# Attention, mixture of experts and feed-forward in one kernel: the gate's logits move out of attention

## The chip, the cores and the metric

The kernel runs on one core of a Trainium2 chip. The metric is the device time of one execution in microseconds (us). TensorE is called PE, its weight loads PEld, VectorE DVE, ScalarE ACT, GpSimd POOL and SyncE SP, as in the profile.

## What is computed

Attention over 4 batches of 8 heads, 576 tokens, head size 64, in a window of 128 tokens with a bias by distance; its output, 2304 tokens of 512, goes through a mixture of 8 experts whose shares come from a gate, and then through a leaky feed-forward layer. The part that matters here:

```python
scores = np.where(mask, scale * (q @ k.T) + bias, -1e9)
attn = exp(scores - max); attn = attn / (sum(attn) + 1e-9); x = attn @ v
logits = x @ w_gate                        # [2304, 512] @ [512, 8]
P = exp(logits - logits.max())             # then 8 rounds of row and column scaling
out += P[:, e:e + 1] * (relu(x @ w1[e]) @ w2[e])
```

## The kernel before

**Attention** works on one pair of heads at a time, 16 pairs (`ITERS`), numbered i; two pairs' buffers alternate (`s`). The 576 query tokens of a pair are 4 tiles of 128 and one of 64, worked on in three groups (`GROUPS`): group 0 is tiles 0 and 1, group 1 tiles 2 and 3, group 2 the tile of 64. Each query tile sees at most two key tiles. For each group:

- PE makes the scores (`scores`, L1116), in fp32: each matmul is two PE instructions.
- DVE adds the bias and takes the row maxima (`bias_scores`, L776).
- ACT takes the exponentials and their row sums (`exponentials`, L541).
- DVE adds a small constant to the sums (L786), takes reciprocals (L788) and scales the rows (L792): `normalise`.
- PE transposes the result (`transpose_p`, L1124), ACT copies it from PSUM (`copy_pt`, L550, L551, L556), PE multiplies with the values (`values`, L1146), and ACT copies the pair's output into `x_raw` (`copy_out`, L562, L563).

The order on each engine is written out by hand in `step`, and the groups of neighbouring pairs are interleaved. For step i:

| Engine | Order in step i |
|---|---|
| PE | scores (i, 2); values (i-1, 1); transposes (i, 0); scores (i+1, 0); values (i-1, 2); transposes (i, 1); scores (i+1, 1); values (i, 0); logits; transposes (i, 2) |
| ACT | copy (i-1, 1); exponentials (i, 1); copy (i-1, 2); copy (i, 0); exponentials (i, 2); output copy (i-1); exponentials (i+1, 0) |
| DVE | bias (i, 2); normalise (i, 1); bias (i+1, 0); normalise (i, 2); bias (i+1, 1); normalise (i+1, 0) |
| POOL | splits of weights and of the first operands, in pieces that wait for given scores (`at`, L382 to L480) |

**Logits** (`logits`, L1152 to L1161): tokens are stationary and the gate's weights, 8 columns, are streamed. The 2304 tokens are 20 parts of 128 or 64 tokens; each takes 4 matmuls (8 instructions), one for each 128 of the 512 input dimensions, accumulated in PSUM. 15 parts are made in steps 4 to 15 of attention (one a step, two in steps 7, 11 and 15), 5 in unit 0.

**Units.** The experts and the feed-forward layer are worked through in granules; each granule is two units (k), of 2 x 256 and 2 x 320 tokens. A unit makes seven products of 6 matmuls each (`product`, L1205 to L1208) into three PSUM banks, which ACT copies and DVE combines, and the down products of tiles of the granule before (`down`). In units 0 and 1 the second unit's first operands are still being cast by ACT (`casts`) and split by DVE (`first_lows`). The logits reach `gate` in unit 1 (`gating`), and the shares are made from them in the units that follow.

Of the kernel before, what the change touches and what calls it, by code (L numbers as in the profile page):

```python
# [5 lines left out]
def attention_moe_ffn(nc, qk_t, v_t, w_gate, w_up, w_down, out, shape):  # L6
# [5 lines left out]
    fp32, f32r = mybir.dt.float32, mybir.dt.float32r  # L12
# [22 lines left out]
    STATS = 2 * SLOTS  # L35
    QT = S // P
# [14 lines left out]
    with ctx:  # L51
# [37 lines left out]
        wg = place("wg", KD * E)  # L89
# [21 lines left out]
        assert at[0] <= acc1_end  # L111
        xs = []
# [11 lines left out]
        bank = [ctx.enter_context(nc.psum_tensor(f"bank{i}", [P, 512], fp32)) for i in range(8)]  # L124
        b_s, b_tail, b_p, b_o = (bank[0:2], bank[3:5]), bank[2], bank[5:7], bank[7]
        b_a, b_b, b_c, b_y, b_m = (bank[0], bank[1]), bank[7], (bank[3], bank[4]), (bank[5], bank[6]), bank[2]
        MAXT, NEGM, COLS = 160, 300, 304
# [9 lines left out]
        wg_ready = sem("wg_ready")  # L137
# [26 lines left out]
        def segments(g, s):  # L164


            sc0, st0 = s * SLOTS * 512, s * STATS
            if g == GROUPS - 1:
                nk = P + TAIL
                return [(hd, QT, (QT - 1) * P, nk, 0, sc0 + 2 * g * 512 + hd * nk, st0 + 4 * g + hd) for hd in range(2)]  # L170
            got = []
            for n in range(2):
                t = 2 * g + n
                nk, c = (P, 0) if t == 0 else (2 * P, (2 * P if g else P) * n)
                for hd in range(2):
                    slot = 2 * g + hd
                    got.append((hd, t, max(t - 1, 0) * P, nk, c, sc0 + slot * 512 + c, st0 + 2 * slot + n))
            return got
# [57 lines left out]
        def logits_at(tile):  # L236

            return tile * E if tile < 16 else 7 * TAIL + (tile - 16) * E
# [10 lines left out]
        def _(sp):  # L249
# [37 lines left out]
            sp.dma_start(wg[:, :].rearrange("p (k e) -> p k e", e=E),  # L287
# [244 lines left out]
        def _(act):  # L532
# [12 lines left out]
            def copy_pt(i, g, s):  # L545
# [76 lines left out]

            def early_copies(k, u):
# [3 lines left out]
                a.activation(t1[:, 0:n], b_a[u][:, 0:n], ACT.Copy).then_inc(t1_copied, 1)  # L627
                act.wait_ge(c_done, 2 * k + 1)
# [24 lines left out]
            def unit(k, u, x2=(), phase=None):  # L653

                n = NU[u]
                early_copies(k, u)
                casts(phase, k, 0)
                copy_u2(k, u)
                act.wait_ge(c11_done, k + 1)
                a.activation(hs_hi[u][:, hidden_part(u, 0, 0)], b_b[:, 0:n], ACT.Relu).then_inc(hi_done, 1)  # L660
                casts(phase, k, 1)
                for tile in x2[0:1]:
                    copy_x2(tile)
                act.wait_ge(c22_done, k + 1)
                a.activation(hs_hi[u][:, hidden_part(u, 1, 1)], b_c[1 - u][:, 0:n], ACT.Relu).then_inc(hi_done, 1)  # L665
                act.wait_ge(c12_done, k + 1)
# [3 lines left out]
                a.activation(hs_hi[u][:, hidden_part(u, 0, 1)], b_a[u][:, 0:n], ACT.Relu).then_inc(hi_done, 1)  # L670
                casts(phase, k, 3)
# [87 lines left out]
        def _(dve):  # L759
            d = nc.vector  # L760

            dve.wait_ge(rel_ready, 1)
# [19 lines left out]
            def normalise(i, g, s):  # L782
                rows = rows_of(g)
                st = slice(s * STATS + 4 * g, s * STATS + 4 * g + len(segments(g, s)))
                dve.wait_ge(exp_done, GROUPS * i + g + 1)
                d.tensor_scalar_add(esum_eps[0:rows, st], esum[0:rows, st], EPS).then_inc(eps_added, 1)  # L786
                dve.wait_ge(eps_added, GROUPS * i + g + 1)
                d.reciprocal(einv[0:rows, st], esum_eps[0:rows, st]).then_inc(inv_done, 1)  # L788
                dve.wait_ge(inv_done, GROUPS * i + g + 1)
# [3 lines left out]
                last.then_inc(normed, 1)  # L793

# [13 lines left out]
            def step(i, s, pair, last=False):  # L808
# [15 lines left out]
            bias_scores(0, 1, 0, 0)  # L824
            normalise(0, 0, 0)
# [82 lines left out]
            def gating(k, point):  # L908
# [3 lines left out]
                if k == 1 and point == 0:  # L912
                    dve.wait_ge(lg_done, 1)
                    split = 16 * E
                    d.tensor_copy(gate[:, 0:split], b_m[:, 0:split]).then_inc(gate_in, 1)
                    d.tensor_copy(gate[:, split:], b_m[:, 7 * TAIL:7 * TAIL + 2 * TILES * E - split]).then_inc(gate_in, 1)
                    dve.wait_ge(gate_in, 2)
# [183 lines left out]
        def _(pe):  # L1101
# [25 lines left out]
            def values(i, g, s, first=False):  # L1127
# [12 lines left out]
                for n, (hd, t, kt, nk, _, b, to) in enumerate(todo):  # L1140
                    if n == len(todo) - 1 and g == 0:

                        pe.wait_ge(normed, GROUPS * i + 3)
# [8 lines left out]
            def logits(b, n):  # L1152

                tile, _, t, rows, p0 = [(tile, *part) for tile in range(TILES) for part in token_parts(tile)
                                        if part[0] == b % 2][n]
                c = logits_at(b // 2 * TILES + tile)
                for kd in range(KD):
                    x = b * HALF + kd * S + t
                    last = m.matmul(b_tail[p0:p0 + rows, c:c + E], x_raw[:, x:x + rows],  # L1159
                                    wg[:, kd * E:(kd + 1) * E], start=kd == 0, stop=kd == KD - 1)  # L1160
                return last  # L1161

# [239 lines left out]
```

## Time and profile before

| | us |
|---|---|
| median of 3 runs | 2050.15 (2049.0 to 2050.66) |
| the profiled execution | 2049.61 |
| its span | 2047.8 |
| end of attention on PE | 137.64 |
| PE busy / PEld busy | 2032.2 / 1815.3 |
| DVE / ACT / POOL busy | 1183.9 / 643.1 / 1167.4 |

The mean granted clock of TensorE is 0.999 of full speed. Some 93% of the span is units; attention is the first 7%. Times in the rows are microseconds from the span's start. In a timeline each row is one instruction or several like it in a row (x8): start, time, engine, line, operation, names, shapes, and in brackets the idle time ahead of it and what ended it. A record of PE, DVE or ACT can overlap the start of the next instruction, so the cost of one in a queue is read from start to start.

### The profile page before, as it was taken

What the parts mean: (1) busy time and instruction counts of PE and PEld (TensorE: products, weight loads), DVE (VectorE), ACT (ScalarE), POOL (GpSimd) and SP (SyncE); (2) the same over time, 40 slices, a digit from 0 to 9 for tenths busy, and PEclk for the clock granted to TensorE, in tenths of its full rate; (3) what the DMA queues carried; (4) which work ended last, traced back from release to release, by engine and by line L of the source; (5) the groups of instructions that cost most, each with busy time, mean ns of one, the idle gap of its engine ahead of it and who ended that gap; (6) DMA issues with size and microseconds to landing.
All of it is one profiled execution on the core that took longest, in us unless ns stands there. A gap on an engine that the chain in (4) does not pass through costs nothing.

```text
span 2047.8 us, 36400 instructions
## 1 busy us (share of the span) xinstructions
PE 2032.2 (99%) x12475; PEld 1815.3 (89%) x12475; DVE 1183.9 (58%) x2708; ACT 643.1 (31%) x1776; POOL 1167.4 (57%) x1451
## 2 busy tenths in 40 slices
PE   8999999999999999999999999999999999999999
PEld 6788999899999899999999999999999989998998
DVE  8876766555555555564555554554554565667666
ACT  8972222222222222233222222222222244334332
POOL 3425556555566565576555566655555575667551
PEclk9999999999999999999999999999999999999999
DMA  5311111111111111111111111111111111111211
GB/s 178 119 66 42 42 42 41 51 41 51 41 41 41 51 41 51 41 37 47 42 52 41 51 41 41 41 51 41 51 41 41 41 41 52 42 52 56 73 42 47
DMA packets 31311, 104.86 MB, mean 51 GB/s; under 512 B 3968, under 2 KB 4480, under 8 KB 31232
## 3 DMA queue, kind: packets, MB, share of 16 engines
q1 hardware_dynamic: 31232, 103.84, 15.1%
q8 instruction: 45, 0.74, 0.1%
q14 instruction: 34, 0.28, 0.0%
HBM read 99.11 MB, written 4.72 MB: 51 GB/s over the span
## 4 chain that ended last, share of the span: by engine, by line
PE 95%; DVE 2%; POOL 1%; ACT 1%; issue 1%; DMA 0%; SPq 0%; ACTq 0%; DVEq 0%; POOLq 0%
PE bank L1227 16%; PE bank L1228 16%; PE bank L1229 16%; PE bank L1205 14%; PE bank L1208 14%; PE bank L1207 14%; PE bank L1146 1%; PE bank L1124 1%; PE bank L1116 1%; PE bank L1159 1%; ACT sc L541 1%; DVE sc L792 1%; POOL up_lo L369 0%; DVE sc L776 0%; PE bank L1243 0%
## 5 line engine op out<-in xcount | busy, mean ns | idle before, releaser
L876 DVE SCALAR_TENSOR_TENSOR acc<-bank,gate,acc 128x512 f32<-128x512 f32 x495 | 371.6, 751 | 573.8 <-PE bank L1229 573.8
L1205 PE MATMUL bank<-x_hi,up_hi 128*128 128x256 f32 (+1 forms) x2240 | 663.3, 296 | 2.0 <-POOL up_lo L369 1.9
L1208 PE MATMUL bank<-x_hi,up_lo 128*128 128x256 f32 (+1 forms) x2240 | 662.9, 296 | 0.0
L1207 PE MATMUL bank<-x_lo,up_hi 128*128 128x256 f32 (+1 forms) x2240 | 662.3, 296 | 0.0
L1228 PE MATMUL bank<-down_lo,hs_hi 128*128 128x512 f32 x1440 | 568.0, 394 | 0.0
L1227 PE MATMUL bank<-down_hi,hs_hi 128*128 128x512 f32 x1440 | 567.5, 394 | 0.4 <-DVE hs_lo L990 0.4
L1229 PE MATMUL bank<-down_hi,hs_lo 128*128 128x512 f32 x1440 | 560.3, 389 | 0.0
L1205 PEld LDWEIGHTS bank<-x_hi,up_hi 128*128 128x128 f32 x2240 | 423.9, 189 | 30.0 <-POOL up_lo L369 2.7
L1207 PEld LDWEIGHTS bank<-x_lo,up_hi 128*128 128x128 f32 x2240 | 423.9, 189 | 23.6
L1208 PEld LDWEIGHTS bank<-x_hi,up_lo 128*128 128x128 f32 x2240 | 423.8, 189 | 0.0
L369 POOL TENSOR_TENSOR up_lo<-stage_up,up_hi 128x256 fp32r<-128x256 f32 x546 | 384.7, 742 | 6.3
L1229 PEld LDWEIGHTS bank<-down_hi,hs_lo 128*128 128x128 f32 x1440 | 270.7, 188 | 61.6
L358 POOL TENSOR_TENSOR stage_up<-stage_up 128x256 f32<-128x256 f32 x78 | 58.3, 748 | 450.0 <-PE bank L1208 450.0
L1227 PEld LDWEIGHTS bank<-down_hi,hs_hi 128*128 128x128 f32 x1440 | 271.7, 189 | 38.1 <-issue 0.8
L1228 PEld LDWEIGHTS bank<-down_lo,hs_hi 128*128 128x128 f32 x1440 | 271.6, 189 | 32.4
L375 POOL CAST down_hi<-stage_down 128x1024 fp32r<-128x1024 f32 x78 | 81.1, 1039 | 263.5 <-PE bank L1229 263.5
L379 POOL TENSOR_TENSOR down_lo<-stage_down,down_hi 128x256 fp32r<-128x256 f32 x312 | 221.4, 743 | 6.3
L984 DVE SCALAR_TENSOR_TENSOR hs_lo<-bank,hs_hi 128x256 fp32r<-128x256 f32 (+1 forms) x512 | 208.9, 448 | 1.5 <-ACT hs_hi L660 1.1
L865 DVE TENSOR_TENSOR acc<-bank,acc 128x512 f32<-128x512 f32 x153 | 105.5, 689 | 111.1 <-PE bank L1229 109.7
L634 ACT ACTIVATE u<-bank 128x256 f32<-128x256 f32 (+1 forms) x160 | 65.7, 411 | 324.7 <-PE bank L1208 324.7
L627 ACT ACTIVATE t<-bank 128x256 f32<-128x256 f32 (+1 forms) x160 | 65.6, 410 | 304.0 <-PE bank L1208 303.7
L665 ACT ACTIVATE hs_hi<-bank 128x256 fp32r<-128x256 f32 (+1 forms) x128 | 52.6, 411 | 340.0 <-DVE bank L968 340.0
(118 smaller groups left out, 1823.1 us busy)
## 6 DMA issues: line engine op xcount, KB each, us to landing
stage_up<-w_up SPq DMA_DIRECT2D x80, 512.0 KB, 3.4
stage_down<-w_down SPq DMA_DIRECT2D x80, 512.0 KB, 3.4
qk<-qk SPq DMA_DIRECT2D x15, 608.0 KB, 3.8
v_nat<-v SPq DMA_DIRECT2D x16, 320.0 KB, 2.9
result<-acc SPq DMA_DIRECT2D x16, 256.0 KB, 2.6
result<-acc SPq DMA_DIRECT2D x4, 128.0 KB, 3.0
qk<-qk SPq DMA_DIRECT2D x2, 128.0 KB, 2.1
qk<-qk SPq DMA_DIRECT2D x1, 192.0 KB, 2.5
```

The costliest lines, as they stand in the source:

```text
L369: last = g.tensor_tensor(up_lo[s][:, part], raw(op), up_hi[s][:, part], ALU.subtract)
L375: g.tensor_copy(down_hi[s][:, :], stage_down[:, :]).then_inc(w_step, 1)
L379: last = g.tensor_tensor(down_lo[s][:, part], stage_down[:, part], down_hi[s][:, part], ALU.subtract)
L865: last = d.tensor_tensor(to, y[:, :], to, ALU.add)
L876: last = d.scalar_tensor_tensor(out=to, in0=y[:, :], scalar=share(g, tile, e), in1=to, op0=ALU.mult, op1=ALU.add)
L984: d.scalar_tensor_tensor(out=hs_lo[u][:, part], in0=of[:, 0:NU[u]], scalar=0.0, in1=hs_hi[u][:, part], op0=ALU.max, op1=ALU.subtract).then ...
L1205: m.matmul(to[:, 0:n], up_hi[s][:, w], x_hi[u][:, x], start=first and c == 0, stop=False, skip_group_check=True)
L1207: m.matmul(to[:, 0:n], up_hi[s][:, w], x_lo[u][:, x], start=False, stop=False, skip_group_check=True)
L1208: last = m.matmul(to[:, 0:n], up_lo[s][:, w], x_hi[u][:, x], start=False, stop=c == 1, skip_group_check=True)
L1227: m.matmul(to[:, :], hs_hi[u][:, h], down_hi[s][:, w], start=f == 0, stop=False)
L1228: m.matmul(to[:, :], hs_hi[u][:, h], down_lo[s][:, w], start=False, stop=False)
L1229: last = m.matmul(to[:, :], hs_lo[u][:, h], down_hi[s][:, w], start=False, stop=f == 1)
```

## The change

The logits leave attention. In units 0 and 1 they are made in 8 pieces of 256 or 320 tokens: the gate's weights, padded with zeros to 32 columns for each 128 input dimensions, are stationary, the tokens are streamed, and the four matmuls of a piece write to four groups of 32 PSUM partitions. ACT copies the piece to SBUF (`lt_sb`), and a second matmul for each part of tokens, with the piece stationary and a 0/1 matrix (`sel`) streamed, adds the four groups and turns the result to tokens by experts. The calls of `logit_tiles` for a piece follow one product after the piece.

In attention, PE's transposes of group 2 move behind values (i-1, 1) of the next step, ahead of the transposes of group 0. DVE makes bias (i+1, 1) before it normalises group 2, and takes the addition and the reciprocal for group 2 and the next pair's group 0 together (`normalise_two`); for this the statistics have new places. ACT copies both heads' transposes of a group with one instruction. On SP the gate weights' DMA waits for POOL's clearing of `wg`.

```diff
@@ names and places @@
+    STAT_AT = ((2, 6, 10), (12, 16, 0))
...
-        wg = place("wg", KD * E)
+        wg = place("wg", KD * P // 4)
+        sel = place("sel", E)
...
+        at[0] = acc1_at
+        lt_sb = [place(f"lt_sb{n}", NU[1]) for n in range(2)]
...
+        def piece(n):
+            return n // 2, NU[0] * (n % 2), NU[n % 2]
@@ SP and POOL @@
+            sp.wait_ge(wg_clear, 1)
+            sp.dma_start(wg[:, :].rearrange("p (k e) -> p k e", e=P // 4)[:, :, 0:E],
                          w_gate.rearrange("(k p) e -> p k e", p=P)).then_inc(wg_ready, 16)
...
+            g.memset(wg[:, :], 0.0).then_inc(wg_clear, 1)
@@ ACT @@
-                    for hd in range(2):
-                        last = a.activation(pt_sb[:, to + hd * 512:to + hd * 512 + n], b_p[hd][:, 0:n], ACT.Copy)
+                    both = [of.rearrange("p (h c) -> p h c", h=2)[:, :, 0:n]
+                            for of in (pt_sb[:, to:to + 1024], bank56[:, :])]
+                    last = a.activation(*both, ACT.Copy)
...
+            def copy_lt(k, *pieces):
+                for n in pieces if isinstance(k, int) else ():
+                    if n // 7 == k:
+                        act.wait_ge(lt_done, n + 1)
+                        cols = piece(n)[2]
+                        a.activation(lt_sb[n % 2][:, 0:cols], b_m[:, LT:LT + cols], ACT.Copy).then_inc(lt_copied, 1)
...
                 a.activation(t1[:, 0:n], b_a[u][:, 0:n], ACT.Copy).then_inc(t1_copied, 1)
+                copy_lt(k, 0, 7)
...
                 early_copies(k, u)
+                copy_lt(k, 1)
                 casts(phase, k, 0)
+                copy_lt(k, 2)
                 copy_u2(k, u)
+                copy_lt(k, 3)
@@ DVE @@
+            d.memset(esum[:, :], 1.0)
...
+            def normalise_two(i, s, n):
+                dve.wait_ge(exp_done, GROUPS * (i + 1) + 1)
+                inverses(P, STAT_AT[s][2], STAT_AT[s][2] + 6, n)
+                scale(2, s)
+                scale(0, 1 - s)
...
                 bias_scores(i, 2, s, pair)
-                normalise(i, 1, s)
+                normalise(i, 1, s, 2 * i + 1)
                 if last:
                     sums(0, 2)
-                if not last:
+                    normalise(i, 2, s, 2 * i + 2)
+                else:
                     bias_scores(i + 1, 0, 1 - s, after)
-                normalise(i, 2, s)
-                if not last:
                     bias_scores(i + 1, 1, 1 - s, after)
-                    normalise(i + 1, 0, 1 - s)
+                    normalise_two(i, s, 2 * i + 2)
+            dve.wait_ge(ident_ready, 1)
+            d.reduce_sum(sel[:, :], ident[:, :].rearrange("p (j c) -> p c j", c=P // 4)[:, 0:E, :], AX.X
+                         ).then_inc(sel_ready, 1)
@@ PE @@
+            def logits(n):
+                b, t, cols = piece(n)
+                if n == 0:
+                    pe.wait_ge(wg_ready, 16)
+                    pe.wait_ge(o_done, ITERS)
                 for kd in range(KD):
+                    rows = slice(kd * P // 4, (kd + 1) * P // 4)
                     x = b * HALF + kd * S + t
+                    last = m.matmul(b_m[rows, LT:LT + cols], wg[:, rows], x_raw[:, x:x + cols], start=True, stop=True)
+                last.then_inc(lt_done, 1)
+            def logit_tiles(n):
...
+                pe.wait_ge(lt_copied, n + 1)
+                for tile in range(TILES):
+                    for half, t0, rows, p0 in token_parts(tile):
+                        if half == b % 2 and t <= t0 < t + cols:
+                            c = (b // 2 * TILES + tile) * E
+                            last = m.matmul(b_m[p0:p0 + rows, c:c + E], lt_sb[n % 2][:, t0 - t:t0 - t + rows],
+                                            sel[:, :], start=True, stop=True)
+            def logit_work(k, point):
...
+                n = 7 * k + point
+                if 0 < n <= 2 * B:
+                    last = logit_tiles(n - 1)
...
+                if n < 2 * B:
+                    logits(n)
...
                 scores(i, 2, s)
                 if not first:
                     values(i - 1, 1, 1 - s)
+                    pe.wait_ge(normed, GROUPS * i)
+                    transpose_p(2, 1 - s)
...
                 values(i, 0, s, first)
-                if i >= KD:
-                    logits(i // KD - 1, i % KD)
-                    if i % KD == KD - 1:
-                        logits(i // KD - 1, KD)
-                transpose_p(2, s)
...
                 product(a_bank, u, s, A11, B11, True).then_inc(a_done, 1)
+                logit_work(k, 0)
...
                 product(c_bank, u, s, S1, T1, True).then_inc(c_done, 1)
-                if isinstance(k, int) and k == 0:
-                    pe.wait_ge(o_done, ITERS)
-                    logits(B - 1, 0)
+                logit_work(k, 1)
```

`logit_work(k, point)` stands behind each of the seven products of units 0 and 1 in the same way, and the old calls of `logits` in unit 0 are gone.

## Rows read from the trace of the kernel before

**Rows 1.** The page, part 1: busy time and share of the span of each engine.

```profile
PE 2032.2 (99%) x12475; PEld 1815.3 (89%) x12475; DVE 1183.9 (58%) x2708; ACT 643.1 (31%) x1776; POOL 1167.4 (57%) x1451
```

**Rows 2.** Timeline of PE, early and late attention: start us, us, engine line op.

```profile
9.97 0.88 PE L1124 MATMUL bank<-ident,sc 128*128 128x128 f32 x6 [2.35 <-DVE sc L792]
...
17.60 0.88 PE L1124 MATMUL bank<-ident,sc 128*128 128x128 f32 x6 [0.42 <-DVE sc L792]
...
129.76 0.88 PE L1124 MATMUL bank<-ident,sc 128*128 128x128 f32 x6
...
134.32 1.62 PE L1159 MATMUL bank<-wg,x_raw 128*128 128x8 f32 x16
...
137.64 0.39 PE L1205 MATMUL bank<-x_hi,up_hi 128*128 128x256 f32 x1
```

**Rows 3.** Timeline of PE, one step of attention with logits.

```profile
56.22 0.88 PE L1124 MATMUL bank<-ident,sc 128*128 128x128 f32 x6
...
57.88 0.60 PE L1146 MATMUL bank<-pt_sb,v_nat 128*64 128x64 f32 x8
58.41 1.09 PE L1124 MATMUL bank<-ident,sc 128*128 128x128 f32 x8
59.43 1.13 PE L1116 MATMUL bank<-qk 64*128 64x256 f32 x8
60.50 0.88 PE L1146 MATMUL bank<-pt_sb,v_nat 128*64 128x128 f32 x12
61.30 1.06 PE L1159 MATMUL bank<-wg,x_raw 128*128 128x8 f32 x8
...
64.08 0.88 PE L1124 MATMUL bank<-ident,sc 128*128 128x128 f32 x6
```

**Rows 4.** Timeline of DVE, the same step.

```profile
59.50 0.54 DVE L792 TENSOR_SCALAR sc<-sc,einv 64x192 f32<-64x192 f32 x2
60.62 0.42 DVE L776 CUSTOM_DVE_ANT_0 sc<-bank,nbias 128x256 f32<-128x256 f32 x1 [0.58 <-issue]
...
62.00 0.17 DVE L786 TENSOR_SCALAR esum_eps<-esum 128x4 f32<-128x4 f32 x1
...
62.42 1.01 DVE L792 TENSOR_SCALAR sc<-sc,einv 128x128 f32<-128x128 f32 x4
63.35 0.35 DVE L776 CUSTOM_DVE_ANT_0 sc<-bank,nbias 64x192 f32<-64x192 f32 x1
```

**Rows 5.** Timeline of ACT, the same step.

```profile
57.13 0.87 ACT L556 ACTIVATE pt_sb<-bank 128x384 f32<-128x384 f32 x2 [0.47 <-PE bank L1124]
```

**Rows 6.** Timelines of POOL and of DVE, early attention.

```profile
15.92 0.83 POOL L399 CAST up_hi<-stage_up 128x768 fp32r<-128x768 f32 x1
...
16.19 1.36 DVE L792 TENSOR_SCALAR sc<-sc,einv 128x128 f32<-128x128 f32 x4
...
31.39 1.64 DVE L792 TENSOR_SCALAR sc<-sc,einv 128x128 f32<-128x128 f32 x4
```

**Rows 7.** Stretches: us, busy by engine, granted clock, DMA share, GB/s.

```profile
103.00:104.00 1.00, 1.00 (x14) 0.78 (x15) 0.35 (x3) 1.00 (x6) 0.25 (x1) 0.88 0.00 0
104.00:105.00 1.00, 1.00 (x12) 1.00 (x10) 0.93 (x8) 0.17 (x2) 0.36 (x1) 0.50 0.27 54
...
107.00:108.00 1.00, 1.00 (x12) 0.67 (x12) 0.02 (x1) 1.00 (x3) 0.00 (x0) 0.91 0.00 0
```

**Rows 8.** Timeline of PE, unit 0: one group of logits.

```profile
139.18 0.96 PE L1159 MATMUL bank<-wg,x_raw 128*128 128x8 f32 x8
139.99 0.36 PE L1205 MATMUL bank<-x_hi,up_hi 128*128 128x256 f32 x1
140.19 0.28 PE L1207 MATMUL bank<-x_lo,up_hi 128*128 128x256 f32 x1
140.31 0.28 PE L1208 MATMUL bank<-x_hi,up_lo 128*128 128x256 f32 x1
```

**Rows 9.** Timeline of ACT: the last output copy of attention.

```profile
138.41 0.21 ACT L563 ACTIVATE x_raw<-bank 128x64 f32<-128x64 f32 x1
```

More of the change, by code:

```diff
@@ L780, in bias_scores, with inverses, scale @@
                 last.then_inc(biased, 1)
-            def normalise(i, g, s):
-                rows = rows_of(g)
[L784 to L789, printed above, removed]
+            def inverses(rows, st0, ends, n):
+                st = slice(st0, ends)
+                d.tensor_scalar_add(esum_eps[0:rows, st], esum[0:rows, st], EPS).then_inc(eps_added, 1)
+                dve.wait_ge(eps_added, n + 1)
+                d.reciprocal(einv[0:rows, st], esum_eps[0:rows, st]).then_inc(inv_done, 1)
+                dve.wait_ge(inv_done, n + 1)
+            def scale(g, s):
+                rows = rows_of(g)
                 for _, _, _, nk, _, c, st in segments(g, s):
@@ L1150, in values @@
                     last.then_inc(pv_done, 1)
[L1152 to L1156, printed above, removed]
+            def logits(n):
[3 more added lines that the diff above has]
+                    pe.wait_ge(o_done, ITERS)
                 for kd in range(KD):
+                    rows = slice(kd * P // 4, (kd + 1) * P // 4)
                     x = b * HALF + kd * S + t
-                    last = m.matmul(b_tail[p0:p0 + rows, c:c + E], x_raw[:, x:x + rows],
-                                    wg[:, kd * E:(kd + 1) * E], start=kd == 0, stop=kd == KD - 1)
-                return last
+                    last = m.matmul(b_m[rows, LT:LT + cols], wg[:, rows], x_raw[:, x:x + cols], start=True, stop=True)
+                last.then_inc(lt_done, 1)
+            def logit_tiles(n):
+                b, t, cols = piece(n)
+                if n == 0:
+                    pe.wait_ge(sel_ready, 1)
+                pe.wait_ge(lt_copied, n + 1)
[5 more added lines that the diff above has]
+                                            sel[:, :], start=True, stop=True)
+                return last
+            def logit_work(k, point):
+                if not isinstance(k, int):
+                    return
+                n = 7 * k + point
+                if 0 < n <= 2 * B:
+                    last = logit_tiles(n - 1)
+                    if n == 2 * B:
+                        last.then_inc(lg_done, 1)
+                if n < 2 * B:
+                    logits(n)
             def step(i, s, first=False, last=False):
@@ L1302, in unit @@
                 product(b_b, u, s, A12, B21, True).then_inc(b_done, 1)
-                if isinstance(k, int) and k == 0:
-                    logits(B - 1, 1)
+                logit_work(k, 2)
                 pe.wait_ge(t1_copied, k + 1)
@@ L1307, in unit @@
                 product(a_bank, u, s, S2, T2, False).then_inc(a_done, 1)
-                if isinstance(k, int) and k == 0:
-                    logits(B - 1, 2)
+                logit_work(k, 3)
                 tile(1)
@@ L1316, in unit @@
                 product(c_bank, u, s, S4, B22, False).then_inc(c_done, 1)
-                if isinstance(k, int) and k == 0:
-                    logits(B - 1, 3)
+                logit_work(k, 4)
                 pe.wait_ge(u2_copied, k + 1)
@@ L1321, in unit @@
                 product(a_bank, u, s, S3, T3, False).then_inc(a_done, 1)
-                if isinstance(k, int) and k == 0:
-                    logits(B - 1, 4).then_inc(lg_done, 1)
+                logit_work(k, 5)
                 tile(2)
```

42 lines of the change are left out of this document (23 added, 19 removed).

## The prediction

> **What bounds the kernel now.** The page comes first: TensorE (PE) is busy for 99% of the span [rows 1], so a change is worth what it takes from PE's own queue or from a wait ahead of it. The change touches only the first 165 us, so the timelines of that stretch are read next, engine by engine. The reader should compare two kinds of step in attention.
>
> In a step without logits PE waits for VectorE (DVE): the first group's transposes begin at 9.97 and then at 17.60, a period of 7.63, with 0.42 us of waiting on the scaling of L792 [rows 2]. From step 4 on PE has the logits as well, and the period is 64.08 - 56.22 = 7.86 without a wait of PE ahead of the transposes [rows 3]. ScalarE (ACT) waits 0.47 us for PE in it [rows 5], DVE 0.58 us [rows 4]. So the 1.0 us of logits per step (61.30, a record of 1.06) stands largely in time that PE would otherwise wait. This is the key to the case: taking them out is worth at most what the next bound allows. After attention the units are bound by PE without gaps, and there every microsecond added to PE counts in full.
>
> **Part 1: logits out of attention.** PE's step falls from 7.86 to about 6.9. ACT occupies 7.86 - 0.47 = 7.39 of the step. These are the floors of the two engines; the edits below decide whether the step reaches them.
>
> **Part 2: the shared reciprocal, and T2 moved.** Before, DVE scaled group 2 while PE made the scores of the next group 1. Now it first adds the bias to those scores, then takes the sum and reciprocal for six columns, scales group 2, and then group 0. That saves one addition and one reciprocal, but puts the scaling of group 2 on a closed chain through DVE and PE. From start to start: transposes and scores of group 0, 57.88 - 56.22 = 1.66; values of group 2, 0.53; transposes of group 1, 1.02 [rows 3]. Scores of group 1 until DVE begins on them, 60.62 - 59.43 = 1.19 [rows 3, 4]. Biasing them, 62.00 - 60.62 = 1.38; addition and reciprocal, 0.42 [rows 4]. Scaling of group 2: 0.54 less the 0.08 by which a following instruction starts before the record ends (62.42 + 1.01 against 63.35), so 0.46 [rows 4]. Scaling of group 0, 1.01 [rows 4], and 0.05 to PE (16.19 + 1.36 = 17.55 against 17.60) [rows 2, 6]. The sum is 7.72 us. The same chain before lacked the 0.46 and made 7.26, hidden under PE's 7.86. So the new step is about 7.7: it gives back only 0.14 of the 1.0 us, and steps without logits before (7.63) gain nothing. The moved transposes of group 2 (half a microsecond) cover themselves: PE has slack ahead of group 0's, and the copy of group 2 waits behind four exponentials on ACT.
>
> **Part 3: GpSimd (POOL) against that chain.** POOL's splits are released by PE's scores. A scaling on DVE stretches while a POOL instruction runs: the 15.92 cast of 0.83 turned 1.01 us into 1.36, and the longest case was 1.64 [rows 6]. Before, the work released by group 2's scores began after DVE's scaling of group 0 was nearly done; now those scores end just before the shared reciprocal, since no logits stand ahead of them. By the code this happens in 11 steps (three in each of two weight splits, five in the first operands). Going by 0.35 with 0.63 as the upper and 0 as the lower end, I take 0.34 each, 3.7 us in all: the casts are as short as the shorter example.
>
> **Attention in sum.** First transposes at 9.97 as before; fifteen steps of 7.72 are 115.8, plus 3.7: the last step begins at 129.5. Before it began at 129.76 [rows 2], although its steps held logits. The last step was 137.64 - 129.76 = 7.9 and loses its 1.55 of logits (a record of 1.62) [rows 2]: 6.35. So attention ends near 135.8 instead of 137.64, **1.8 less**. Of the old time, 1.7 was not work: the granted clock fell to 0.50 (1.2 GHz) in step 11, behind two parts of logits (16 instructions of 8 columns); clocks of 0.88, 0.50 three times and 0.91 in five 1-us slices lose 0.12 + 1.5 + 0.09 = 1.7 us [rows 7]. I expect no such drop now. If it comes anyway attention is a tie. The copy of both heads in one ACT instruction saves at most 0.1 per copy and ACT is not on the chain: zero, unless ACT becomes the bound.
>
> **Part 4: logits in units 0 and 1.** Eight pieces, each of four fp32 matmuls (each is two PE instructions) of 256 or 320 columns, into four groups of 32 output rows. No such matmul is in the trace. The nearest is the scores: four 256-column fp32 matmuls of alternating heads take 59.43 to 60.50, that is 1.06 [rows 3], with the two halves of a head pair overlapping. The two instructions of one matmul use the same part of the array, so only neighbours overlap; I take the same price: 1.06 for 256 and 1.06 x 320/256, or 1.3, for 320. Four of each: 9.4 us. Ends: if all four groups stream together, an instruction costs the 0.066 of the values matmuls (0.53 for 8) [rows 3], so 8 x 8 x 0.066 = 4.2; if nothing overlaps, twice the price, 18.8.
>
> The second step, with the copied logits as weights, has twenty fp32 matmuls of 8 columns; that is as many as unit 0 runs now, in five groups of 0.81 (139.18 to 139.99) or less [rows 8]. They replace each other: 0. Each insertion also delays the product behind it (0.20 between its first two matmuls in place of 0.12) [rows 8]; 16 insertions (8 pieces, 8 second steps) instead of 5 add 11 x 0.08 = 0.9. The first piece waits for the last output copy, which ended at 138.41 + 0.21 = 138.62 [rows 9], one microsecond after the unit's start, while only one product (0.7) stands ahead of it now instead of two: 0.3. The eight copies on ACT (about 0.4 each) stand in its idle time, behind a product of 0.7 or more on PE; a late one would stop PE in the second step. I count zero, with up to 1 us as its upper end. **Sum of the units: 9.4 + 0.9 + 0.3 = +10.6.**
>
> GpSimd's extra memset, DVE's memset and its small reduction stand ahead of the first scores, which wait for a DMA; the gate weights' DMA now waits on SyncE for that memset, behind nine loads. I count zero, at most 0.3. One gate copy instead of two on DVE in unit 1: 0, it is not on PE's path.
>
> **The sum.** 2049.61 - 1.8 + 10.6 = 2058.4 us against the profiled execution, whose time lies 0.5 below the median of the three runs shown. Later granules are untouched. I round down to 2058, since more of the open bounds lie below.
>
> **The rivals.**
> - **Four groups at once (2053).** The pieces cost 4.2 instead of 9.4: 2058.4 - 5.2 = 2053.2. For it: values matmuls of two output halves cost 0.066 per instruction, near what issuing alone might cost. Against: the scores' price shows no more than two streams. The Trainium skill, page "TensorE: Matmul & The Clock Gate", section "Measured speedup vs the span model", gives 2.38x for three column groups; no run here shows it yet, and by it the pieces would come out near this rival. Chance 0.22.
> - **POOL misses the chain (2055).** Its work falls between the scalings, as in most steps of before: 3.7 less, 2054.7. Chance 0.10.
> - **ACT, not the DVE-PE chain, bounds the step (not slower).** If the bias of group 1's scores isn't late, steps fall to 7.39 less the 0.1 or so of the single copy, 7.3: fifteen are 109.5, the stage ends at 125.9, 11.7 less, and the time is 2049.6 - 11.7 + 10.6 = 2048.5; with the first rival too, 2043. It decides where the closed chain is under 7.3, that is 0.4 shorter than I sum it; the 7.63 period of before, with ACT hardly waiting, speaks against it. Chance 0.08.
> - **A clock drop (2060 or more).** Waits now stand in every step, and 32-column groups may count as little work. Each drop costs 1.7 as in rows 7; one gives 2060.1, two 2061.8. Against: the fall of before followed step 11 with its double logits, not the early steps with their waits. Chance 0.10.
> - The forecast, 0.50.
>
> **How the numbers follow.** A measurement can tell about 0.2%, 4.1 us, from no change: beyond 2054.3 it is slower, under 2046.1 faster. Slower: 0.57 of the 0.60 that the forecast and the clock rival hold, and 0.13 of the 0.32 of the first two rivals, which stand near the bound: 0.70. Faster needs the ACT rival together with cheap pieces: 0.06. Within: 0.24. The range takes in the first two rivals and one or two clock drops: 2050.5 to 2063.5; it leaves out the ACT rival, and pieces without overlap (2068).
>
> **What the profile would show.** Right: periods of 7.7 to 8.3 between first transposes, PE waiting there for the scaling, DVE waiting for group 1's scores, no clock of 0.5 in attention, and pieces of 1.06 and 1.3 in unit 0, which grows by some 8 us. Wrong: periods near 7.3 with ACT without gaps; pieces of 0.6; PE waiting in the units on the logit copies.

## The result, and the profile after

The changed kernel takes 2055.43 us (median of 10 runs, 2054.31 to 2056.06), the one before, run beside it, 2050.24 (10 runs, 2049.0 to 2051.53): a ratio of 1.0026, 95% interval [1.0018, 1.0034]. It is slower by 5.2 us; the forecast was 2058, between 2050.5 and 2063.5. The profiled execution took 2056.06 with a span of 2053.5, 5.7 more than the span of before. Part 1 of its page, beside [rows 1]:

```profile
PE 2029.4 (99%) x12419; PEld 1805.1 (88%) x12419; DVE 1175.9 (57%) x2679; ACT 647.2 (32%) x1752; POOL 1167.0 (57%) x1452
```

PE is busy for 2.8 us *less* than before, and yet the span is longer: in attention, waiting has come in for work. The waits of PE, from the same profile (what waited, on what, us in total, times, longest), show where. The single line in the second block is from the same view of the kernel before:

```profile
PE bank L1164 <- DVE sc L820: 9.9, 22, 2.3
PE bank L1156 <- DMA qk<-qk: 4.4, 2, 3.5
PE bank L1183 <- ACT pt_sb L566: 3.9, 14, 0.3
```

```profile
PE bank L1124 <- DVE sc L792: 4.9, 7, 2.3
```

The kernel before has 4.9 us in 7 waits for the scaling and 0.8 us in 2 for ACT's copies; now it is 9.9 us in 22 and 3.9 us in 14. The timeline of PE in attention, after, beside [rows 2, 3]:

```profile
3.51 1.65 PE L1156 MATMUL bank<-qk 64*128 64x128 f32 x8 [3.51 <-DMA qk<-qk]
6.03 2.72 PE L1156 MATMUL bank<-qk 64*128 64x256 f32 x12 [0.87 <-DMA qk<-qk]
11.02 1.54 PE L1164 MATMUL bank<-ident,sc 128*128 128x128 f32 x6 [2.27 <-DVE sc L820]
12.49 1.65 PE L1156 MATMUL bank<-qk 64*128 64x128 f32 x8
14.07 1.97 PE L1164 MATMUL bank<-ident,sc 128*128 128x128 f32 x8
...
20.83 0.88 PE L1164 MATMUL bank<-ident,sc 128*128 128x128 f32 x6 [0.48 <-DVE sc L820]
...
44.63 0.88 PE L1164 MATMUL bank<-ident,sc 128*128 128x128 f32 x6 [0.30 <-DVE sc L820]
...
46.29 0.60 PE L1183 MATMUL bank<-pt_sb,v_nat 128*64 128x64 f32 x8
46.82 1.09 PE L1164 MATMUL bank<-ident,sc 128*128 128x128 f32 x8
47.84 1.13 PE L1156 MATMUL bank<-qk 64*128 64x256 f32 x8
...
50.59 1.09 PE L1183 MATMUL bank<-pt_sb,v_nat 128*64 128x128 f32 x16 [0.28 <-ACT pt_sb L566]
...
52.35 0.88 PE L1164 MATMUL bank<-ident,sc 128*128 128x128 f32 x6 [0.29 <-DVE sc L820]
...
60.41 0.88 PE L1164 MATMUL bank<-ident,sc 128*128 128x128 f32 x6 [0.47 <-DVE sc L820]
...
137.24 0.39 PE L1266 MATMUL bank<-x_hi,up_hi 128*128 128x256 f32 x1
```

A clean step (44.63 to 52.35) lasts 7.72. PE waits twice in it: 0.28 for ACT's copy at 50.59, and 0.29 for DVE at 52.35, ahead of the next first transposes. 60.41 - 52.35 = 8.06 is a step stretched by POOL. The first (20.83 - 11.02 = 9.81) is far longer, with records of 1.54, 1.65 and 1.97 where the same instructions take 0.88, 0.93 and 1.09 elsewhere. Attention ends at 137.24 instead of 137.64. DVE in the clean and in the stretched step, beside [rows 4]:

```profile
49.03 0.42 DVE L802 CUSTOM_DVE_ANT_0 sc<-bank,nbias 128x256 f32<-128x256 f32 x1 [1.30 <-issue]
...
50.41 0.17 DVE L811 TENSOR_SCALAR esum_eps<-esum 128x6 f32<-128x6 f32 x1
...
50.84 1.46 DVE L820 TENSOR_SCALAR sc<-sc,einv 64x192 f32<-64x192 f32 x6
...
58.13 0.23 DVE L811 TENSOR_SCALAR esum_eps<-esum 128x6 f32<-128x6 f32 x1
...
58.62 1.74 DVE L820 TENSOR_SCALAR sc<-sc,einv 64x192 f32<-64x192 f32 x6
```

The six scalings (two of group 2, four of group 0) follow the six-column addition and reciprocal: 1.46 in the clean step, 1.74 in the other. POOL has no instruction beside the first; beside the second it has:

```profile
58.27 0.83 POOL L408 CAST up_hi<-stage_up 128x768 fp32r<-128x768 f32 x1
```

Unit 0 on PE, beside [rows 8], and the first matmul of the shares' work on `lmax` and `ones`, which both kernels have. The second block has that matmul in the timeline of before:

```profile
138.37 0.64 PE L1198 MATMUL bank<-x_raw,wg 128*32 128x256 f32 x8 [0.16 <-ACT x_raw L573]
138.94 0.38 PE L1266 MATMUL bank<-x_hi,up_hi 128*128 128x256 f32 x1
...
139.75 0.51 PE L1211 MATMUL bank<-sel,lt_sb 128*128 128x8 f32 x4
140.19 0.75 PE L1198 MATMUL bank<-x_raw,wg 128*32 128x320 f32 x8
140.86 0.39 PE L1266 MATMUL bank<-x_hi,up_hi 128*128 128x256 f32 x1
...
141.67 0.72 PE L1211 MATMUL bank<-sel,lt_sb 128*128 128x8 f32 x6
...
170.67 0.38 PE L1320 MATMUL bank<-lmax,ones 1*128 1x1 f32 x2
```

```profile
165.03 0.38 PE L1259 MATMUL bank<-lmax,ones 1*128 1x1 f32 x2
```

A piece of 256 columns holds PE from 138.37 to 138.94, 0.57; one of 320 from 140.19 to 140.86, 0.67. From the start of the unit to that last matmul it is 170.67 - 137.24 = 33.43, before 165.03 - 137.64 = 27.39: **the units cost 6.0 more, attention gives back 0.4**. Together that is 5.6 of the span's 5.7.

### The profile page after: what moved, and what is told of

It is laid out like the page before. It is cut to its first block, busy times and chain, and to the rows that moved or that the text cites. A ratio compares the mean times of both kernels' runs of the same rounds, so it can differ in the third digit from the quotient of the medians.

```text
span 2053.5 us, 36262 instructions
## 1 busy us (share of the span) xinstructions
PE 2029.4 (99%) x12419; PEld 1805.1 (88%) x12419; DVE 1175.9 (57%) x2679; ACT 647.2 (32%) x1752; POOL 1167.0 (57%) x1452
## 4 chain that ended last, share of the span: by engine, by line
PE 91%; DVE 5%; issue 2%; POOL 1%; ACT 0%; DMA 0%; DVEq 0%; SPq 0%; POOLq 0%
PE bank L1288 16%; PE bank L1289 16%; PE bank L1290 16%; PE bank L1266 14%; PE bank L1269 14%; PE bank L1268 14%; DVE sc L802 2%; DVE sc L820 2%; POOL up_lo L378 0%; PE bank L1304 0%; POOL x_lo L499 0%; DVE einv L813 0%; DVE neg_max L802 0%; PE bank L1198 0%; PE bank L1211 0%
```

## The experiments

The main theory after the result: attention's step is held by the closed chain through DVE and PE, lengthened by POOL where it meets the shared reciprocal, and the units' cost is PE's own work. The rivals put the time in PE's order, in ACT's copies or in the clock of the first steps; each expectation says what its theories give for its run. The first four runs are set against 2049.98 us for the kernel before, the next four (from the mixed kernel on) against 2050.13, the three after these against 2050.00, and the last against 2049.41.

**The changed kernel again**, the ground for the others.

> The changed kernel itself, for the beginning of the span. Its profile had a late load (VectorE waited 1.60 us for the second scores) and records of twice the length from 11 to 16 us, and began its second step at 20.83 instead of 17.6. Theory A (chance): this beginning comes from the time a load lands and varies by execution; here the second step begins between 17.8 and 21, median near 2055.4. Theory B (the change): the later memory clearing or the wait on SyncE delays the loads; the second step begins at 20.8 again.

2054.62 us (1.0023 [1.0014, 1.0032]). Chain steps of 7.72 as above; unit 0 begins at 136.08, because the first transposes come at 10.56 instead of 11.02 and the first period is 9.12 instead of 9.81. The second step begins at 19.68, inside the 17.8 to 21 of Theory A. The second `qk` load held PE for 0.38 here, for 0.87 in the profile above, and not at all in the profiles of the five other runs built on the changed kernel, so the late load is chance and not the change. Windows of this run (us; busy of PE, PEld, DVE, ACT, POOL; granted clock; DMA):

```profile
11.00:12.00 1.00, 1.00 (x11) 0.83 (x10) 0.67 (x5) 0.81 (x3) 0.00 (x0) 0.68 1.10 393
12.00:13.00 1.00, 1.00 (x7) 0.35 (x5) 0.89 (x4) 1.00 (x5) 0.00 (x0) 0.50 0.63 247
13.00:14.00 1.00, 1.00 (x7) 1.00 (x6) 0.92 (x8) 0.16 (x2) 0.88 (x2) 0.50 0.09 34
14.00:15.00 1.00, 1.00 (x7) 0.68 (x7) 0.27 (x2) 0.69 (x4) 0.53 (x1) 0.62 0.00 0
```

The clock falls to 0.50 here, which is 1.2 GHz; the four windows lose 0.32 + 0.50 + 0.50 + 0.38 = 1.7 us of PE's time.

**DVE's old order alone.** The logits stay in the units, the transposes of group 2 stay moved, and DVE no longer shares the reciprocal.

```diff
                     bias_scores(i + 1, 0, 1 - s, after)
+                normalise(i, 2, s, 3 * i + 2)
+                if not last:
                     bias_scores(i + 1, 1, 1 - s, after)
-                    normalise_two(i, s, 2 * i + 2)
+                    normalise(i + 1, 0, 1 - s, 3 * i + 3)
```

> The changed kernel with VectorE's old order (group 2 scaled before the bias of the next group 1; each group has its own reciprocal). Theory A (closed chain through the shared reciprocal): the period of the first transposes falls from 7.72 to 7.3-7.6 in steps without GpSimd's pieces beside them, attention is 3 us shorter (2 to 4), median near 2052.4. Theory B (the sharing is neutral, and attention is bound by ScalarE or the values' copies): periods stay at 7.7, median within 0.5 us of the changed kernel, or above it, since two instructions per step come back.

2050.43 us (1.0002 [0.9993, 1.0011]), 4.2 under the changed kernel. Its timeline of PE: a step of 63.30 - 55.82 = 7.48, without a wait ahead of the first transposes (the x10 holds the four transposes of group 2 and the six of group 0). Attention ends 4.7 earlier than in the run above: 0.6 from earlier first transposes, 0.5 from the first period, 3.6 from the steps after it.

```profile
55.82 1.36 PE L1165 MATMUL bank<-ident,sc 64*128 64x64 f32 x10
...
63.30 1.36 PE L1165 MATMUL bank<-ident,sc 64*128 64x64 f32 x10
...
131.35 0.39 PE L1267 MATMUL bank<-x_hi,up_hi 128*128 128x256 f32 x1
```

So the shared reciprocal, with the order on DVE that it needs, costs 4.2 us; with both gone, the move of the logits is a tie. The two were not tried apart: the sharing can't be had while group 2 is scaled ahead of the bias, but the order could be without the sharing.

**The whole old order of attention, logits in the units.**

```diff
-                    transpose_p(2, 1 - s)
...
                 values(i, 0, s, first)
+                transpose_p(2, s)
```

(beside the edit of DVE above, with the old wait of group 0's last transpose)

> The changed kernel with the whole old order in attention (VectorE's, and the transposes of group 2 back behind the values of group 0), logits in the units. This is attention without logits. Theory A: periods of 7.3 to 7.6 with 7.9 at most where GpSimd interferes, 3.5 to 4.5 us under the changed kernel, near 2051.3; and so the logits cost the old attention only 0.3 us a step. Theory B (logits cost their full 1.0 us per step): 9 to 10 us shorter, near 2046.

2051.55 us (1.0007 [0.9998, 1.0016]). Unit 0 starts at 133.63, against 137.64 with the logits. From the second first transposes on (20.07 here, 17.60 before), attention takes 113.56 instead of 120.04, 6.5 less; 1.7 of that is the clock drop of before [rows 7], which leaves 4.8 us for 15 parts of logits, or 0.32 each. That is Theory A, and far from the 1.0 of Theory B. The total is 3.1 under the changed kernel, where 3.5 to 4.5 was expected. Moving the transposes of group 2, which separates this run from the one above, gains 1.1 by the medians, though the two intervals overlap; in the profiles 1.5 of the 2.3 between the two starts of unit 0 stands ahead of the second first transposes (20.07 against 18.60), so how much the move itself is worth stays open.

**The kernel before with the shared reciprocal and the moved transposes**, its logits left in attention.

```diff
+    STAT_AT = ((2, 6, 10), (12, 16, 0))
...
+                    normalise_two(i, s, 2 * i + 2)
...
+                    pe.wait_ge(normed, GROUPS * i)
+                    transpose_p(2, 1 - s)
```

> The kernel before with only the shared reciprocal and the transposes of group 2 moved; logits stay where they were. Theory A: the chain of 7.72 and the PE work of 7.86 are both near the bound and each stop by GpSimd adds to it: 1.5 to 4 us slower than before, near 2053. Theory B (sharing saves VectorE work and costs nothing): within 0.5 us of before.

2053.82 us (1.0019 [1.0010, 1.0029]): +3.8 us without any change of the logits. Unit 0 starts at 140.71, 3.1 after the kernel before. The edit moves the transposes as well, so the 3.8 is the price of both together.

**The mixed kernel**: the kernel before with only the last batch's logits, which stood in unit 0 already, in the new form, and one copy of the gate.

```diff
-                    logits(B - 1, 0)
+                    last_logits(0)
...
-                    logits(B - 1, 1)
+                    last_logit_tiles(0)
+                    last_logits(1)
...
-                    logits(B - 1, 2)
+                    last_logit_tiles(1).then_inc(lg_done, 1)
```

> The kernel before, with only the last batch's logits (the five parts of unit 0) made in the new form: two pieces with the gate's weights stationary, two second steps. The rest of the logits stays in attention. In the changed kernel a piece of 256 and one of 320 take about 0.6 and 0.7 us and their second steps 0.44 and 0.65, 2.4 in all, against 3.8 for five parts. Theory A (a part in attention costs 0.3 us, one in unit 0 costs all of it): 1.0 to 1.5 us faster than before, near 2049.0. Theory B (switching between the forms and the copies on ScalarE eat it): within 0.4 us of before.

2048.57 us (0.9994 [0.9985, 1.0003]), the lowest median of all. The interval holds 1, so that it beats the kernel before is not shown; that it beats the changed one is (the intervals against before lie apart). Seven of its 11 times lie under the lowest of the 27 of before (2049.03), so a small gain is likely.

```profile
138.72 0.64 PE L1183 MATMUL bank<-x_raw,wg 128*32 128x256 f32 x8
139.29 0.38 PE L1242 MATMUL bank<-x_hi,up_hi 128*128 128x256 f32 x1
...
140.54 0.74 PE L1183 MATMUL bank<-x_raw,wg 128*32 128x320 f32 x8
141.22 0.39 PE L1242 MATMUL bank<-x_hi,up_hi 128*128 128x256 f32 x1
...
144.99 0.38 PE L1242 MATMUL bank<-x_hi,up_hi 128*128 128x256 f32 x1 [0.53 <-DVE bank L983]
```

Two pieces (0.57 and 0.68) and two second steps take the place of five groups of logits. From unit 0's start to the same matmul as above it is 26.77 instead of 27.39, although PE now waits 0.53 for DVE's combining of a bank, and 0.27 for `hs_lo`: a shorter PE meets the next bound here too. So the units give 0.6 and not the 1.0 to 1.5 of Theory A. Of the 1.2 between the two spans (2046.6 and 2047.8) the other half lies ahead of unit 0 (137.09 against 137.64), where PE's code is the same and the start and the place of the clock drop differ (from 10 to 14 us here, at 104 in the profile of before).

**One column group.** The four matmuls of a piece accumulate in the same 32 output rows; the second step contracts over 32.

```diff
-                    last = m.matmul(b_m[rows, LT:LT + cols], wg[:, rows], x_raw[:, x:x + cols], start=True, stop=True)
+                    last = m.matmul(b_m[0:32, LT:LT + cols], wg[:, rows], x_raw[:, x:x + cols], start=kd == 0, stop=kd == KD - 1)
```

> The changed kernel with the four matmuls of a logits piece accumulated in one group of 32 output rows instead of four; the second step reads 32 rows. Theory A (the four groups stream at the same time): a piece rises from 0.6 and 0.7 us to the full time of eight instructions one behind another, 1.7 and 2.1 (256 or 320 columns at twice the 0.12 us that an fp32r matmul of 256 columns takes), 10 us slower in all. Theory B (each instruction needs one pass at 0.12 and the order matters little): a piece stays under 1.1 us, at most 3 us slower.

2066.79 us (4 runs; 1.0081 [1.0066, 1.0097]), 12.2 over the changed kernel.

```profile
136.73 1.89 PE L1198 MATMUL bank<-x_raw,wg 128*32 128x256 f32 x8 [0.16 <-ACT x_raw L573]
138.54 0.39 PE L1266 MATMUL bank<-x_hi,up_hi 128*128 128x256 f32 x1
...
139.99 2.34 PE L1198 MATMUL bank<-x_raw,wg 128*32 128x320 f32 x8
142.26 0.39 PE L1266 MATMUL bank<-x_hi,up_hi 128*128 128x256 f32 x1
```

A piece holds PE for 138.54 - 136.73 = 1.81 and 142.26 - 139.99 = 2.27, against 0.57 and 0.67: ratios of 3.2 and 3.4, and 4 x (1.81 + 2.27 - 0.57 - 0.67) = 11.4 us of the 12.2. The four groups stream at once. The edit also makes the matmuls accumulate, and what this alone costs wasn't tried; but overlap there is in any case, since eight of the products' instructions of 256 columns, which stand 0.12 apart [rows 8], would take 0.96, and a piece takes 0.57.

**POOL released later.** The pieces that waited for group 2's scores wait for the next group's.

```diff
-                pool.wait_ge(s_done, GROUPS * i + group + 1)
+                pool.wait_ge(s_done, GROUPS * i + group + (2 if group == 2 else 1))
```

> The changed kernel, where GpSimd's pieces of work that were released by group 2's scores wait for the next group's scores. Theory A (their beginning beside the shared reciprocal stops VectorE's scalings): all periods are 7.72, attention 1.5 to 2.5 us shorter, near 2053.4. Theory B (it is only moved to another scaling on the chain): within 0.5 us of the changed kernel.

2052.20 us (1.0009 [1.0000, 1.0018]), 2.4 under the changed kernel. First transposes in its timeline of PE:

```profile
26.45 0.88 PE L1164 MATMUL bank<-ident,sc 128*128 128x128 f32 x6 [0.26 <-DVE sc L820]
...
57.38 0.87 PE L1164 MATMUL bank<-ident,sc 128*128 128x128 f32 x6 [0.35 <-DVE sc L820]
```

All steps after those at the start of attention, from 26.45 on, are 7.71 to 7.77 long. The cast that stood across the shared reciprocal, 2.14 ahead of the next first transposes (58.27 against 60.41), now begins 1.81 behind them (59.19 against 57.38), as its timeline of POOL has it:

```profile
59.19 0.85 POOL L408 CAST up_hi<-stage_up 128x768 fp32r<-128x768 f32 x1 [3.61 <-PE bank L1156]
```

**Two copies instead of one.**

```diff
-                    both = [of.rearrange("p (h c) -> p h c", h=2)[:, :, 0:n]
-                            for of in (pt_sb[:, to:to + 1024], bank56[:, :])]
-                    last = a.activation(*both, ACT.Copy)
+                    for hd in range(2):
+                        last = a.activation(pt_sb[:, to + hd * 512:to + hd * 512 + n], b_p[hd][:, 0:n], ACT.Copy)
```

> The changed kernel with two copies, one for each head, instead of one. Theory A (ScalarE is not on the chain): no difference, within 0.4 us of the changed kernel. Theory B (ScalarE bounds the step): 15 steps of two copies at 0.05 to 0.1 more, 1.5 to 3 us slower.

2054.81 us (1.0021 [1.0012, 1.0030]), as the changed kernel: the single copy is worth nothing while DVE holds the step.

**Filling PE's idle start**: the kernel before, with ten fp32 matmuls of `ident` whose results nobody reads.

```diff
             pe.wait_ge(ident_ready, 1)
+            fill(2)
             scores(0, 0, 0, first=True)
             scores(0, 1, 0, first=True)
+            fill(8)
```

> The kernel before with 10 fp32 matmuls of the identity with itself (128 columns, results unused) on TensorE: 2 ahead of the first scores, 8 behind the second scores, where it waited 2.35 us for the first scaling. Theory C (the half clock from about 10 to 15 us, seen in nine of the ten profiles so far, follows the idle time at the beginning and costs 1.5 to 2.5 us): the records of the first two transposes groups take 0.88 and 1.09 and the kernel is 1 to 2 us faster than before, near 2048.7. Theory D (it does not hang on TensorE's work there, or the added work only delays the first scores): same or up to 1 us slower.

2048.88 us (0.9997 [0.9988, 1.0006]), 1.1 under the kernel before. No clock drop in the profiled run, neither at the start nor at 104, which has a span of 2046.5; the times fall into two heaps, six of 2047.8 to 2048.9 and five of 2049.9 to 2051.6. The interval holds 1; not settled by this run.

**The mixed kernel with the moved transposes and the single copy**, and the same **with filling**. The edits are those shown above.

> The mix kernel (last batch's logits in the new form, the others in attention, own reciprocals) with the transposes of group 2 moved as in the change and one copy for both heads. Theory A: old_dve against old_attention gave 1.1 us for the move where TensorE has slack; here TensorE bounds the steps with logits, so only the four steps without them and the last one gain: 0.2 to 1.0 us under the mix kernel, near 2048.0. Theory B: the moved wait on the scaling of group 2 stands ahead of group 0's transposes and costs something: up to 0.5 us over it.

2050.13 us (1.0001 [0.9992, 1.0010]), 1.6 over the mixed kernel. Theory A expected 0.2 to 1.0 under it: where the logits stand in attention the move doesn't help. But its profiled run had the first load 0.6 late, so that part of the 1.6 can be the start.

> mix_moved with the same 10 filling matmuls as before_fill. If theory C holds the gains add up: 2046.5 (3.5 us under the kernel before); if not, as mix_moved.

2048.89 us (0.9994 [0.9985, 1.0003]), 1.1 under the kernel before where 3.5 was expected, and 1.2 under the run without filling. The profiled run was the slowest of the 11 (2052.29). The filling matmuls have the length of half clock themselves in it (3.78 us for 16 instructions, against 2.05 in the kernel before with filling), and the granted clock falls again at the end of attention (0.61, 0.50, 0.50 and 0.69 in the windows from 138 to 142, around the start of unit 0).

**The mixed kernel with filling.**

> The kernel that was the best so far (the one before, with the last batch's logits in unit 0 in the new form and a single gate copy; 1.6 us under before) with ten filling fp32 matmuls in PE's idle start. Theory C (half-clock stretches of 3 us in the first period cost 1.5 to 2 us in most runs, and filling prevents them in some of them): a median 0.5 to 1.2 us under that kernel, so 2.1 to 2.8 us under before, near 2047.6 (ratio 0.9988), with two clusters of times about 2 us apart. Theory D (the filling does nothing for the median, the 1.2 us it seemed to give twice is spread): 1.6 us under before, 2048.5. In both, unit 0 up to the product's wait on the late first operands is as long as without the filling (26.8 us).

2049.16 us (11 runs, 2047.47 to 2050.36; before 2049.41; 0.9996 [0.9987, 1.0005]). Against its own group that is 0.25 under before, and the mixed kernel without filling had 1.6: a gain for the median from the filling is not shown. The profiled run, at 2050.36 the slowest of the 11, shows two ways in which the filling pays less than expected. The first is in its timeline of PE:

```profile
7.38 2.82 PE L1229 MATMUL bank<-ident 128*128 128x128 f32 x16
10.13 0.59 PE L1131 MATMUL bank<-qk 64*128 64x192 f32 x4
...
13.54 1.09 PE L1139 MATMUL bank<-ident,sc 128*128 128x128 f32 x8 [1.16 <-DVE sc L806]
```

The filling took 2.82 us, where the same 16 instructions took 2.05 in the kernel before with filling, so that the scores of group 2 came at 10.13, and the second transposes waited 1.16 for DVE. The second is that the drop isn't gone: it stands at 104 to 108, as in the profile of before [rows 7].

```profile
105.00:106.00 1.00, 1.00 (x10) 0.62 (x8) 0.49 (x4) 0.59 (x4) 0.46 (x1) 0.50 0.00 0
```

This slice of 1 us and its neighbours (0.80 ahead of it, 0.50 in the two behind it) lose 0.2 + 3 x 0.5 = 1.7 us. The chances of Theory C as a way to gain time fall with this: a drop kept from attention's start can come later. That a drop stands in the first period without filling, as it says, holds.

## Why the prediction was right, and where its sizes were off

**What bounds the kernel, Parts 1 and 2: right.** The floor of PE's step fell, though not quite to 6.9: in the clean step it is 7.72 - 0.28 - 0.29 = 7.15 without the two waits. The closed chain took over. Its sum was 7.72, and the clean steps are 7.72 (eight of the fourteen periods after the first are within 0.01 of it, the other six are those of Part 3). By terms, in the step from 44.63: values begin 1.66 later, transposes of group 1 0.53 later, scores 1.02; DVE begins 49.03 - 47.84 = 1.19 after them, needs 1.38 for the bias, 0.43 for addition and reciprocal, 1.46 for the scaling, and PE begins 0.05 behind it. Nothing of the 1.0 us per step of logits came back beyond 0.14. The run with DVE's old order (-4.2) and the one with the sharing in the old kernel (+3.8) show both sides.

**Part 3, POOL against the chain: right in kind, too large.** Forecast 11 steps of 0.34, 3.7 us. The periods show 0.21, 0.43, 0.34, 0.22, 0.43 and 0.44 in six steps, 2.1 us, and the run with POOL released later took 2.4 away. The size per meeting was right (0.34 in the mean of the six); the term that failed is the count of 11. The two weight splits meet the chain three times each, as forecast: five of these meetings are in the six periods above, one is in the first period (cast at 18.70, scaling at 19.04 and 1.74 long). Of the five steps with the first operands only one is longer, 8.16. In the others the cast ends early in the scaling, and the scaling keeps its 1.46:

```profile
90.02 0.61 POOL L444 CAST x_hi<-x_raw 128x512 fp32r<-128x512 f32 x1
```

```profile
90.42 1.46 DVE L820 TENSOR_SCALAR sc<-sc,einv 64x192 f32<-64x192 f32 x6
```

The stretched scaling of 1.74 instead of 1.46 shows the meeting itself: the cast began at 58.27, ahead of the scaling at 58.62, and DVE lost 0.28 there and 0.06 in the addition. The Trainium skill, page "SBUF — State Buffer", section "SBUF: two separate sides", calls the port pair that VectorE and GpSimd share an exclusive lock: where a VectorE instruction runs in a two-port mode, or has two inputs in SBUF, the later one of the two engines is blocked until the other's instruction ends. Whether these scalings run in such a mode no run here shows. By that rule alone the scaling would have been held for up to 58.27 + 0.83 - 58.62 = 0.48; the measured stretch is 0.28, in the same direction and smaller. The one beside the cast of 90.02 would have been held for 0.21 and shows nothing. Records on POOL are rough, so the differences aren't explained.

**Attention in sum: -1.8 forecast, -0.4 measured.** Against the forecast of 135.8: the first transposes came 1.05 later (the second load of `qk` landed 0.87 late), the first period was 9.81 - 7.72 = 2.1 longer (half clock, and the one meeting with POOL in it), POOL took 1.6 less, the last step 0.1 less; 135.8 + 1.05 + 2.1 - 1.6 - 0.1 = 137.25. The step that failed is "I expect no such drop now": the drop of step 11 went away, and another stood in the first period, worth about the same. That "no clock of 0.5 in attention" came true in the windows is no confirmation, since the records have the length of half clock.

**Part 4, the pieces: the term that failed.** Forecast 9.4 with "only neighbours overlap"; measured 4 x (0.57 + 0.67) = 5.0, near the lower end of 4.2. The rival "four groups at once" was right on this term, and "pieces of 0.6", which the prediction gives as a sign of being wrong, is what the profile shows. The nearest row was the wrong one: scores show two streams because they have only two, the heads' halves. An instruction of 256 columns costs 1.81 / 8 = 0.226 in one group and 0.57 / 8 = 0.071 in four; scores with two halves cost 0.133 [rows 3], between the two. By the Trainium skill, page "TensorE: Matmul & The Clock Gate", section "Measured speedup vs the span model", three column groups gave 2.38x; the 3.2x and 3.4x of four groups here agree with its direction, in fp32, with the accumulation mixed in. Dividing the forecast's price without overlap by that figure gives 18.8 / 2.38 = 7.9 us, an estimate, which lies nearer the 9.4 of the forecast than the rival's 4.2; so the page's figure for three groups, which the prediction puts near that rival, doesn't by itself give the 5.0 measured.

The rest of the units: the second steps take 4.5 us together (0.44, 0.65, 0.44, 0.75 and so on, start to start), the five groups of logits before 3.8, so the swap put at 0 cost 0.7. The delays of products, 16 by the forecast, are 9, since a second step and the next piece stand together: 9 x 0.10 less 5 x 0.08 = 0.5 instead of 0.9. The wait for the output copy was 0.16 instead of 0.3. ACT's copies cost nothing. 5.0 + 0.7 + 0.5 + 0.16 = 6.4 beside the 6.0 measured (before had a wait of 0.16 that is gone; 0.2 is unaccounted for).

**The total.** Forecast -1.8 + 10.6 = +8.8; measured -0.4 + 6.0 = +5.6. Sign and range were right; the two errors of size that decide stand against each other, pieces 4.4 less and attention 1.4 more. That the median came within 2.6 of the forecast is in part luck: with the pieces as cheap as they were and attention as forecast, the sum would have given 2054.0, and the start of the span, which the prediction took over unchanged from the profile of before, brought 3.1 more, of which POOL's missing meetings hid 1.6.

## What to carry to other kernels

Work that stands in an engine's waiting time is free there; before moving it, sum the closed chain through the other engines, since that is what the step becomes. Sharing a small instruction between an urgent and a less urgent piece of work saves some 0.4 us of VectorE a step (the addition and reciprocal of rows 4) and puts the less urgent piece on the chain: here it cost 4.2 us in all. Small-output matmuls are worth spreading over different column groups (0.57 us for a piece instead of 1.81), and a price for them must come from a row with the same number of groups, not from the nearest shape.

## What the runs showed of the hardware

**The clock in the first steps.** In ten of the eleven profiles without filling the granted clock stood at 0.50 (1.2 GHz), or like records had that length, for some 3 us between 10 and 17 us, after PE had idled for 2.3 to 2.6 us ahead of the first transposes. The first period was then 8.65 to 10.4 us long; without the drop it was 7.63 in the profile of before. Idling of this length alone doesn't decide it: the profile of before idled 2.35 us too, and has its drop at 104 [rows 7], where PE was busy. Filling the idle time moved the drop more than it removed it: the mixed kernel with filling has it at 104 to 108, the one with the moved transposes has half-clock lengths in the filling itself and a drop at 138 to 142, and only the profile of the kernel before with filling has none. So 13 of the 14 profiles hold such a stretch, and what decides its place is open. The first scores, at 3.51 in the changed kernel, have the length of half clock too (1.65, later 0.93).

In the profiled run of the changed kernel the windows read 1.00 through the stretch while the records had the length of half clock (12.49: 1.65 instead of 0.93), so a mean clock of 1.0 doesn't exclude a drop; the length of like records does.

```profile
12.00:13.00 1.00, 1.00 (x7) 0.67 (x7) 0.96 (x5) 0.41 (x1) 0.00 (x0) 1.00 0.85 332
```

**Loads at the start.** The second `qk` load held PE for 0.87, 0.38 or not at all in executions of nearly the same start. With the clock this makes the start a matter of 2 us between executions, about as much as most of the edits here are worth, and is why a single profile can't be set against another without taking the first 20 us, and any later drop, out.
